# Attention, gated convolution FFN and mixing FFN in one program: first tiles' last products moved behind their partners, and four reorderings around them

## The reference

```python
# attention, per batch and head; cum = cumsum(max(s, 0))
scores = q @ k.T / 8 + minimum(-(cum[:, None] - cum[None, :]), 0), causal
attn = exp(scores - max); attn /= attn.sum() + 1e-9
x = concat_heads(attn @ v)                       # 576 x 512
# first FFN: w_in 512 x 1024, conv_w 3 taps along the sequence, w_out 1024 x 512
h = maximum(x @ w_in, 0)
conv = conv_w[0]*h[s-1] + conv_w[1]*h[s] + conv_w[2]*h[s+1]
x1 = (h * sigmoid(conv)) @ w_out
# mixing: U 576 x 32, V 32 x 576; second FFN: w_ch1 512 x 2048, w_ch2 2048 x 512
u = x1 + (x1.T @ U @ V).T
out = u + maximum(u @ w_ch1, 0) @ w_ch2
```

## Time and profile before

| | us |
|---|---|
| median of 3 runs (lowest, highest) | 910.75 (907.56, 912.88) |
| the profiled execution, whole | 910.62 |
| its span, first to last instruction | 908.8 |

### The profile page before, as it was taken

The page is one execution under the profiler, slowest core; times in us unless marked ns, Lnnn a source line. Parts: engine busy times, 40 slices in busy tenths (PEclk is TensorE's granted clock), DMA queues, the critical chain, the costliest instruction groups (busy, mean ns, idle before and its releaser), DMA issues.

```text
span 908.8 us, 15655 instructions
## 1 busy us (share of the span) xinstructions
PE 861.6 (95%) x6184; PEld 809.2 (89%) x6184; DVE 468.5 (52%) x984; ACT 372.5 (41%) x709; POOL 50.6 (6%) x105
## 2 busy tenths in 40 slices
PE   4888898989999999999999999999999999999998
PEld 3666888879998999889998999988999999999998
DVE  6788694464445934555344871455323761442222
ACT  2777675554425634544332653444221431221110
POOL 3021000000000000000000000000000000000000
PEclk9999998989999999999999999999999999999999
DMA  7686945636663557336545454435444444274441
GB/s 162 164 228 157 305 141 189 222 73 199 214 209 104 188 167 259 127 106 212 180 152 177 129 172 145 134 100 184 146 145 169 141 174 150 94 240 182 150 175 53
DMA packets 64396, 150.36 MB, mean 165 GB/s; under 512 B 30026, under 2 KB 44362, under 8 KB 51780
## 3 DMA queue, kind: packets, MB, share of 16 engines
q1 hardware_dynamic: 61252, 144.50, 49.4%
q0 software_dynamic: 3072, 4.87, 2.1%
HBM read 119.15 MB, written 30.11 MB: 164 GB/s over the span
## 4 chain that ended last, share of the span: by engine, by line
PE 66%; DVE 13%; issue 10%; ACT 5%; DMA 4%; POOL 1%; SPq 1%; DVEq 0%; ACTq 0%; POOLq 0%
PE psum L1190 18%; PE psum L1192 18%; PE psum L1191 17%; PE psum L1169 5%; DVE work L958 2%; DVE psum L899 2%; PE psum L1116 2%; DVE work L961 2%; DMA few_scratch<-few 2%; PE psum L1148 2%; PE psum L1146 2%; DMA spread_out<-few_scratch 2%; DVE work L956 1%; ACT work L746 1%; DVE ybuf L973 1%
## 5 line engine op out<-in xcount | busy, mean ns | idle before, releaser
L1190 PE MATMUL psum<-r_hl,ring 128*128 128x288 f32 x512 | 153.6, 300 | 3.2 <-DVE r_hl L1001 1.7
L1190 PE MATMUL psum<-uu_hl,ring 128*128 128x288 f32 x512 | 153.2, 299 | 1.5 <-DVE r_hl L1001 1.5
L1192 PE MATMUL psum<-r_hl,ring 128*128 128x288 f32 x512 | 151.2, 295 | 0.0
L1191 PE MATMUL psum<-r_hl,ring 128*128 128x288 f32 x512 | 151.1, 295 | 0.0
L1192 PE MATMUL psum<-uu_hl,ring 128*128 128x288 f32 x512 | 151.0, 295 | 0.0
L1191 PE MATMUL psum<-uu_hl,ring 128*128 128x288 f32 x512 | 150.9, 295 | 0.0
L783 ACT ACTIVATE r_hl<-psum 128x288 fp32r<-128x288 f32 x128 | 52.5, 411 | 188.1 <-PE psum L1192 188.0
L1001 DVE SCALAR_TENSOR_TENSOR r_hl<-psum,r_hl 128x288 fp32r<-128x288 f32 x128 | 58.5, 458 | 134.7 <-ACT r_hl L783 134.6
L1169 PE MATMUL psum<-probs,va 128*65 128x320 f32 (+4 forms) x448 | 109.6, 364 | 6.5 <-ACT probs L694 6.3
L899 DVE CUSTOM_DVE_ANT_0 psum<-psum,key_late 128x512 f32<-128x512 f32 (+4 forms) x160 | 84.9, 564 | 57.1 <-PE psum L1116 56.8
L1190 PEld LDWEIGHTS psum<-r_hl,ring 128*128 128x128 f32 x512 | 96.6, 189 | 5.5 <-DVE u_acc L1013 2.7
(11 more groups left out here) (101 smaller groups left out, 1626.6 us busy)
## 6 DMA issues: line engine op xcount, KB each, us to landing
ring<-w_scratch SPq DMA_DIRECT2D x74, 1024.0 KB, 4.9
w_scratch<-ring SPq DMA_DIRECT2D x24, 1024.0 KB, 6.1
kq_raw<-in_kq_t SPq DMA_DIRECT2D x64, 288.0 KB, 5.0
stage<-in_w_ch SPq DMA_DIRECT2D x16, 512.0 KB, 4.7
spread_out<-few_scratch POOLq DMA_DIRECT2D x32, 144.0 KB, 3.2
...
```

The source lines that it names most:

```text
L1190: pe.matmul(o, hi, m_hi, start=start, stop=False)
L1191: pe.matmul(o, hi, m_lo, start=False, stop=False)
L1192: return pe.matmul(o, lo, m_hi, start=False, stop=stop)
```

## The change

- `first_products`: in the first pair of w_in, of w_out and of the second FFN's up (unit 0), half 0 does all k-tiles but the last, then half 1 does all but its last, then half 0's last (which waits for the last low part), then half 1's last.
- `turn_at`: head 3 of batch 1 has its turning of maxima (`max_transpose`, `max_to_row`) at step 4, not 3, that is behind the first w_out item of batch 0.
- `EVICT_LATE`: in heads whose step 4 holds turn, rank or mix items, ACT takes the head's result out at the step's end, not at its beginning.
- `key_low` and `query_low` one step later in batches 1 to 3.
- `X_SPLIT`, `NORMALISE`: in batches 1 to 3 pairs 0 and 1 are normalised and split later in the batch.
- `invert_few` of the last pair: for batches 1 to 3 at the end of the last attention step (h=7, g=4), not in the next batch's first step or as END's item 2.
- `rank` waits for each turned tile by itself, in the order of their turning.
- `middle_tap`: in the last batch the convolution's middle tap is made by ACT instead of DVE.

```diff
--- before.py
+++ after.py
@@ -253,6 +253,11 @@
         MAXIMA = [{0: (0, 1), 1: (2,)}, {0: (0,), 1: (1,), 2: (2,)}]
         TURN = [3, 3]
 
+        def turn_at(a, h):
+            return TURN[a > 0] + ((a, h) == (1, 3))
         COPIED = H + 2
         ATT_STEPS = [(h, g) for h in range(H) for g in range(GROUPS)]
 
@@ -334,7 +339,7 @@
                   for a in range(1, B)}
         PLAN = {a: spread(BESIDE[a], len(ATT_STEPS) - 6 * (a == 1), 6 * (a == 1), a == 1) for a in BESIDE}
         END = order(B - 1, second(B - 2, UNITS // 2, UNITS)) + flat(second(B - 1, 0, UNITS))
-        END_INVERT, END_NORMALISE, END_SPLIT = 2, 5, {0: NPAIR - 2, 6: NPAIR - 1}
+        END_NORMALISE, END_SPLIT = 5, {0: NPAIR - 2, 6: NPAIR - 1}
         SEQ = [item for a in range(1, B) for item in BESIDE[a]] + END
         AT = {item: at for at, item in enumerate(SEQ)}
 
@@ -433,11 +438,14 @@
         STEPS = [(a, h, g) for a in PLAN for h, g in ATT_STEPS]
         STEP_BEFORE = dict(zip(STEPS[1:], [items for plan in PLAN.values() for items in plan]))
 
-        X_SPLIT = [{(5, 0): 0, (7, 0): 1}, {(4, 0): 0, (6, 0): 1}]
+        EVICT_LATE = {(a, h) for a in PLAN for h in range(H - 1)
+                      if any(x[0] in ("turn", "rank", "mix") for x in PLAN[a][GROUPS * h + GROUPS - 1])}
+        X_SPLIT = [{(5, 0): 0, (7, 0): 1}, {(5, 0): 0, (7, 0): 1}]
         X_SPLIT_LAST = [{}, {(0, 2): (NPAIR - 2,), (1, 0): (NPAIR - 1,)}, {(0, 0): (NPAIR - 2,), (0, 2): (NPAIR - 1,)}]
 
-        NORMALISE = [(4, 6), (3, 5, 7)]
-        INVERT_LAST = [(0, 1), (0, 0)]
+        NORMALISE = [{(4, 2): 0, (6, 2): 1}, {(4, 1): 0, (6, 1): 1, (7, 3): 2}]
         NORMALISE_LAST = [(0, 4), (0, 1)]
 
         def multiplied(eng, item):
@@ -711,12 +719,12 @@
                     act.activation(x_hl[0][:, pair, :], x_raw[:, pair, :], ACT.Copy).then_inc(xh_done.sem, 1)
 
                 def attention_step(a, h, g):
-                    if g == TURN[a > 0]:
+                    if g == turn_at(a, h):
                         max_to_row(a, h + 1)
                     if g == 3 and not a:
                         prepare_keys(a, h + 2)
                         prepare_queries(a, h + 2)
-                    if g == 4:
+                    if g == 4 and (a, h) not in EVICT_LATE:
                         evict_head(a, h)
                     for c in {0: (0, 1), 1: (2,), 2: (3,)}.get(g, ()):
                         exponentials(a, h, c)
@@ -730,6 +738,8 @@
                         prepare_keys(a, h + 2)
                     if g == 3:
                         prepare_queries(a, h + 2)
+                    if g == 4 and (a, h) in EVICT_LATE:
+                        evict_head(a, h)
 
                 def hidden(b, f, half):
                     mm_wi.wait(act, b, 2 * f + half + 1)
@@ -737,6 +747,13 @@
                     act.activation(hid[:, f % 2, 1 + half * HALF:1 + (half + 1) * HALF],
                                    half_at("wi", b, 0, f, half), ACT.Relu)\
                        .then_inc(relu.sem, 1)
+                def middle_tap(b, f):
+                    m = b * FT + f
+                    relu.wait(act, b, 2 * f + 2)
+                    yl_done.wait(act, m - 2)
+                    act.activation(conv[f % 2], hid[:, f % 2, 1:S + 1], ACT.Copy, scale=cw[:, 1, f:f + 1]).then_inc(cv.sem, 1)
 
                 def gate(b, f):
                     cv.wait(act, b * FT + f)
@@ -812,6 +829,8 @@
                     kind, b, unit, i, half = item
                     if kind == "wi":
                         hidden(b, i, half)
+                        if half and b == B - 1:
+                            middle_tap(b, i)
                         if i and not half:
                             gate(b, i - 1)
                     if kind == "gated":
@@ -836,6 +855,7 @@
                     if g == 1 and h in WEIGHTS_HEADS:
                         weights_high(MADE[WEIGHTS_HEADS.index(h)])
                 act.wait_ge(s_hid, 1)
+                act.wait_ge(cw_in, 48)
                 bodies(body_step, ffn_step, then)
                 follow(PLAN[B - 1][-1][-1])
                 for x, item in enumerate(END):
@@ -934,16 +954,18 @@
                         query_low(a, h + 2)
                     if g == 3 and h in (2, 4, 6):
                         invert_few(a, h // 2 - 1)
-                    if g == 2 + (a > 0) and h in NORMALISE[a > 0]:
-                        normalise_few(a, NORMALISE[a > 0].index(h))
-                    if g == 2 and a:
+                    if (h, g) in NORMALISE[a > 0]:
+                        normalise_few(a, NORMALISE[a > 0][h, g])
+                    if g == 3 and a:
                         key_low(a, h + 2)
-                    if g == 3 and a:
+                    if g == 4 and a:
                         query_low(a, h + 2)
                     if (a, h, g) == (1, 0, 1):
                         normalise_few(0, NPAIR - 2)
-                    if a and (h, g) == INVERT_LAST[a > 1]:
-                        invert_few(a - 1, NPAIR - 1)
+                    if (a, h, g) == (1, 0, 1):
+                        invert_few(0, NPAIR - 1)
+                    if a and (h, g) == (H - 1, 4):
+                        invert_few(a, NPAIR - 1)
                     if a and (h, g) == NORMALISE_LAST[a > 1]:
                         normalise_few(a - 1, NPAIR - 1)
 
@@ -953,7 +975,8 @@
                     yl_done.wait(dve, m - 2)
                     if f < 2 and b:
                         acc.wait(dve, b - 1, 2 * f + 2)
-                    dve.tensor_scalar(conv[i], hid[:, i, 1:S + 1], cw[:, 1, f:f + 1], None, ALU.mult).then_inc(cv.sem, 1)
+                    if b < B - 1:
+                        dve.tensor_scalar(conv[i], hid[:, i, 1:S + 1], cw[:, 1, f:f + 1], None, ALU.mult).then_inc(cv.sem, 1)
                     cv.wait(dve, m, 1)
                     dve.scalar_tensor_tensor(out=conv[i], in0=hid[:, i, 0:S], scalar=cw[:, 0, f:f + 1], in1=conv[i],
                                              op0=ALU.mult, op1=ALU.add).then_inc(cv.sem, 1)
@@ -1074,8 +1097,6 @@
                 dve.wait_ge(cw_in, 48)
                 bodies(attention_step, ffn_step, then)
                 for x, item in enumerate(END):
-                    if x == END_INVERT:
-                        invert_few(B - 1, NPAIR - 1)
                     if x == END_NORMALISE:
                         normalise_few(B - 1, NPAIR - 1)
                     if x in END_SPLIT:
@@ -1178,7 +1199,7 @@
                         max_transpose(a, h + 1)
                     if g >= 1:
                         values(a, h, g - 1)
-                    if g == TURN[1] and a:
+                    if g == turn_at(a, h) and a:
                         max_transpose(a, h + 1)
                     if g in (1, 2):
                         scores(a, h, g + 1)
@@ -1214,26 +1235,37 @@
                     if kind == "down":
                         acc.wait(pe, b, NTH[item] + 1)
 
-                def products(item, tiles, m_hi, m_lo, ready=None):
+                def products(item, tiles, m_hi, m_lo, ready=None, ks=None):
 
                     half = item[-1]
                     hi, lo = weights(item)
-                    for k in range(tiles):
+                    for k in ks or range(tiles):
                         if ready:
                             ready(k)
                         mm = three(half_at(*item), hi[:, k, :], lo[:, k, :], m_hi[:, k, cols(half)], m_lo[:, k, cols(half)],
                                    k == 0, k == tiles - 1)
                     return mm
 
+                def first_products(item, tiles, m_hi, m_lo, ready):
+                    if item[-1] == 0:
+                        other = (*item[:-1], 1)
+                        products(item, tiles, m_hi, m_lo, ready, range(tiles - 1))
+                        if BEFORE[other]:
+                            evicted(BEFORE[other])
+                        products(other, tiles, m_hi, m_lo, None, range(tiles - 1))
+                    return products(item, tiles, m_hi, m_lo, ready, range(tiles - 1, tiles))
                 def wi(item):
                     _, b, _, f, half = item
                     x_ready = lambda k: xl_done.wait(pe, b * NPAIR + k)
-                    products(item, KT, *x_hl, x_ready if f == 0 and half == 0 else None).then_inc(mm_wi.sem, 1)
+                    (products(item, KT, *x_hl) if f else first_products(item, KT, *x_hl, x_ready)).then_inc(mm_wi.sem, 1)
 
                 def wo(item):
                     _, b, _, d, half = item
                     y_ready = lambda k: yl_done.wait(pe, b * FT + k)
-                    products(item, FT, *y_hl, y_ready if d == 0 and half == 0 else None).then_inc(mm_wo.sem, 1)
+                    (products(item, FT, *y_hl) if d else first_products(item, FT, *y_hl, y_ready)).then_inc(mm_wo.sem, 1)
 
                 def turn(b, t, half):
 
@@ -1247,12 +1279,16 @@
 
                 def rank(b, half):
 
-                    x1l.wait(pe, b)
```

(15 more changed lines are left out.)

## The result

| | before | changed |
|---|---|---|
| median (lowest, highest), us | 910.06 (907.56, 912.88), 6 runs | 899.29 (897.76, 901.21), 6 runs |
| the profiled execution, whole | 910.62 | 898.22 |
| its span | 908.8 | 896.4 |
| its mean granted clock of PE | 0.992 | 0.996 |

The ratio is 0.9882 with a 95% interval of 0.9855 to 0.9909: the changed kernel is 1.2% faster. The forecast was 898.0 with a range of 893.5 to 903.5.

A forecast was written before the change was run, and what follows sets the result against it. PE, busy 95% of the span, was taken as the bound, so gains come from its waits: 5.8 + 1.4 + 2.0 + 1.5 + 1.95 = 12.65 us off 910.6 gives 898, range 893.5 to 903.5.

The forecast's parts named there:

- First w_out, 5.8: Batch 0's first w_out pair: turning behind 42 matmuls at full clock, ending at 144.6 instead of 150.4, 5.8 us gained.
- the rival in which the first w_out gains nothing: Last `y_low` as late as PE was, clock still falls: 5.8 shrinks to 1, total 906, chance 5%.
- Net 0.2 earlier: Batch 0's w_in: covered stall of 0.96 less 0.76 for a query's low part, so the last `y_low` comes 0.2 us earlier.
- my 0.76: A query's low part moved into DVE's dense w_in stretch: 0.76 us cost, also taken off twice in later batches.
- Rank, 1.4: Batch 0's rank at 182.56: its 1.7 us wait for the last two turned tiles shrinks, 1.4 us gained.
- Heads of w_in, 1.34, 1.83 and 1.3: Stalls for x's last low part at the w_in heads of batches 1, 2 and the last one go entirely.
- Late eviction, 1.4 and 0.46: Beside the next batches: relu no longer behind head 3's evict, removing PE stalls of 1.4 and 0.46 us.
- End, 0.65: Last w_in: tap on ACT cuts the period from 3.65 to 3.5, taking 0.65 us off the stall at 739.50.
- The 2.6 us for the 6.9 us at 139.5: First low-clock stretch, in batch 0's first w_out item: 2.6 us lost on 24 matmuls, counted as regained.
- two clock rivals: Clock falls elsewhere or the first stretch stays: 901, 12%. Second low stretch goes too: 895, 13%.
- the slower rival, SP's queue: Raw key and query loads delay ring loads queued behind: 0.7 for each of 23 heads gives 914, chance 4%.
- DVE's backlog: Rival: gains at the heads of stages return as longer waits for the maxima, 902, chance 15%.

The follow-up runs named there:

- e1: The kernel before with only head 3's turning of maxima moved behind the first w_out item: 910.28 us, ratio 1.0026.
- e3: The kernel before with both the moved turning of head 3's maxima and `first_products`, no other edit: 903.45 us, ratio 0.9946.
- e6: The changed kernel with the heads' results taken out at the beginning of step 4 everywhere, as before: 901.09 us, ratio 0.9932.
- e2: The kernel before with `first_products` alone: 907.82 us, ratio 0.9982.
- e5: The changed kernel with low parts of keys and queries back at their old steps: 899.44 us, ratio 0.9907.
- e11: e10 with low parts back at old steps in heads 0 to 2 of batch 1 and for head 0's query in batches 2 and 3: 894.31 us.
- e8: The changed kernel with rank waiting once for all turned tiles, in the old order: 898.66 us, ratio 0.9898.
- e7: The changed kernel with the last pair's inversion back where it was before: 905.05 us, ratio 0.9955.
- e4: The changed kernel with the last batch's middle tap back on DVE: 899.28 us, ratio 0.9893.
- e10: The changed kernel with turning of maxima of heads (2,1) and (3,1) also at step 4, and the middle tap back on DVE: 901.94 us, ratio 0.9919.
- e12: The changed kernel word for word, run again on the same chip as three of its variants: 900.57 us, ratio 0.9913.

## Why the prediction was right, and where it was not

Set against the ledger, the sum of 12.65 stands so (first relu rows to last, profiled against profiled, 12.4 us):

| stretch | predicted gain, terms | measured |
|---|---|---|
| up to batch 0's third relu | 0.96 | 1.5 |
| D | -0.76 | -2.0 |
| A | (5.8 - 0.2) + 1.4 + 1.34 = 8.34 | 8.7 |
| B | 1.4 - 0.76 + 1.83 = 2.47 | 2.5 |
| C | 0.46 - 0.76 + 1.3 = 1.0 | 2.0 |
| end | 0.65 | -0.2 |

The 8.7 in A agree with 8.34 by some luck. A of before has 10.24 us more of low clock, at 0.39 worth 4.0 us, and the sum had only the 2.6 of the first stretch; so the code brought 4.7 where the sum had 5.7. By places (start of the pair's, the rank's last matmul): 5.8 up to the end of the first w_out pair (150.36 and 145.06; the sum 5.6), 1.1 more up to the rank's end (187.52 and 181.16; the sum 1.4), 1.8 more up to batch 1's w_in (the sum 1.34), of which 1.3 are the second low stretch, half as long.

**First w_out, 5.8.** Right as a mechanism and as a number: 42 matmuls unbroken, the last `y_low` done at 143.1 (forecast 142.5), half 1's end at 145.2 (forecast 144.6), full clock there. The absolute times fit by some luck, since the trace was ahead by 1.5 us at the third relu and then lost 2.0 in D. e1 and e3 show that neither move does it alone; the rival in which the first w_out gains nothing is what e1 measured.

**Low parts in batch 0's w_in: mis-sized.** The step that failed is "Net 0.2 earlier", 0.96 for the covered stall less 0.76 for one query's low part. The 0.96 came: from PE's wait for the exponentials in front of w_in (92.38 in before, 92.75 in e6, both at full clock behind it) to the third relu are 9.29 us before and 8.28 in e6, and D is the same 33.2 in before and in e2, so PE's lead is kept. But the low parts cost 2.0 in D, not 0.76 (e5, e11 and every run of the table by its setting). D holds four of them in either kernel, but behind 110, where DVE hardly pauses, stand three now (112.2, 128.1, 131.0) and two before (123.2, 128.7): that is my 0.76. The rest is where they stand: PE waits 1.0 us longer for the maxima of 120.03, which the move put behind more work of DVE. I had priced the length of the piece and not who waits behind it; which of the three costs how much was not tested. What helped the sum is that the later step brings 1.8 back in A, of which I had only the 0.6 of the key's low part. In batches 2 and 3, where I took off 0.76 twice, that cost came, 1.0 and 0.8 in the w_in stretches (e5), but not as the longer wait for maxima that I named: at 304.27 it is 0.64, as at 311.45 before, and the 0.81 at 295.96 is new. What I had at nothing, the other low parts, brings 0.9 and 0.7 behind them, and so B and C come out the same with either setting.

**Rank, 1.4.** The size is about right, 1.0 to 1.3 from the late eviction (e6) and 0.4 from the waits by tile (e8) when each is undone, 1.1 for the whole change between the w_out pair and the rank's end. My "exponentials come some 0.3 later" is the new wait at 189.43; it is 0.4 longer than the mix's wait that it stands in for. That wait of 1.20 (195.41), like the 1.55 at 92.38, contradicts my sentence that the stalls left out are shorter than 1.1 us and that the change touches none: with the low parts in their old places it is back (1.21 in e5).

**Heads of w_in, 1.34, 1.83 and 1.3.** The waits went, but the reason given was half wrong. I wrote that nine matmuls lie in front as well, and costed the evictions of half 1's bank at nothing. e2, e3 and e7 show that in batches 1 and 2 `first_products` alone only changes the name of the wait (in the last it took 1.16 off C), and that without the earlier inversion the changed kernel is 5.8 us slower. What removes the wait is that DVE no longer stands long in front of its evictions: it waits 0.27 and 0.49 for the spread DMA of the last pair, where it was 2.26 and 2.75 before and is 2.17 and 2.74 in e7. In the last batch the reciprocal stands 17.1 us ahead of the third relu, 14.9 before: 2.2 sooner, not 3.5, and enough.

**Late eviction, 1.4 and 0.46.** B's size came (1.50 in e6) but only a third of it where I put it: at 368.57 e6 waits 0.85, the changed kernel still 0.33 at 367.45; e6 loses 0.4 more behind that and 0.6 at the head of batch 2's w_in. C was too small (1.07). I had priced only the one stall that named it, at 591.09; e6 has two in that stretch, 0.30 and 0.25 of idle time or 0.46 and 0.41 as stalls (starts 582.82 and 624.58).

**End, 0.65: wrong in sign.** The loop was drawn rightly, its link from ACT to DVE was too short. ACT's groups by line from 694 to 740 (mean ns is the second number), then the loop in ACT's and DVE's timelines:

```profile
L756 ACT ACTIVATE work<-hid,cw 128x576 f32<-128x576 f32 x8 | 6.2, 778 | 0.3
L763 ACT ACTIVATE work<-work 128x576 f32<-128x576 f32 x8 | 5.5, 686 | 8.1 <-DVE work L984 8.1
```

```profile
711.52 0.69 ACT L763 ACTIVATE work<-work 128x576 f32<-128x576 f32 x1 [0.96 <-DVE work L984]
712.11 0.40 ACT L747 ACTIVATE hid<-psum 128x288 f32<-128x288 f32 x1
712.54 0.78 ACT L756 ACTIVATE work<-hid,cw 128x576 f32<-128x576 f32 x1
```

```profile
709.82 0.82 DVE L981 SCALAR_TENSOR_TENSOR work<-hid,cw,work 128x576 f32<-128x576 f32 x1 [0.45 <-ACT work L756]
...
713.45 0.82 DVE L981 SCALAR_TENSOR_TENSOR work<-hid,cw,work 128x576 f32<-128x576 f32 x1 [0.45 <-ACT work L756]
```

Tanh to relu 0.59, relu to tap 0.43, tap to DVE's next tap 0.91 (713.45 - 712.54: 0.78 and 0.13 of hand-over), two taps 1.70: 3.63, where I had 0.69 for the tap's link and 3.5 in sum. The period before was 3.65. So nothing is won a tile, and the first tile's tap comes 0.4 later (0.91 for 0.51): e4, e10 and e11 all have 0.2 to 0.25 less at the end. The Trainium skill (ScalarE: Activation LUTs, What ACT_TABLE_LOAD costs) says that each per-partition operand of an activation adds about 93 ns; the rows agree, 778 against 686 ns, and I had not used it.

**The clock.** The 2.6 us for the 6.9 us at 139.5 agree with what A shows for the same code, 0.39 us for each us at the lower level. By the Trainium skill (TensorE: Matmul & The Clock Gate, HAM oscillation) it would be half of the length, an estimate of 3.4 for 6.83; the runs give 2.66. That part of such a stretch is idle or paced by others is my reading and was not tested. Of the two clock rivals each came half true: the second low stretch shrank by half, and a short one stood at 90.5. The Trainium skill's other rule (the same page, A second HAM failure mode), that frequent short idles suffice, fits the place, for behind 100 us no idle time longer than 1.6 us precedes the fall at 189.5; but the same short idles did not always bring a fall, see the last section.

**Medians and one execution.** The pair of traces differs by 12.4 us, the medians by 10.8; the trace had a head start by chance. Its wait for the exponentials in front of w_in stands at 90.28, in before at 92.38, in all fourteen traces at 90.3 to 93.9 (e12, the same kernel, at 91.86), with no edit that explains these. Of the 2.1 us, with the stall's 1.0 added, the low clock at 90.5 took 1.5 back, which leaves the 1.5 of the first row. The forecast's 898.0 lies within the changed kernel's runs, but its errors (D and the end against the head start, the clock in A and C) cancelled in it. No matmul waits for a ring load (PE's table of waits has no row for one), so the slower rival, SP's queue, did not come; DVE's backlog came as the 2.0 in D and the 1.0 and 0.8 in the next two w_in stretches. The later normalising of pairs 0 and 1 and the reordered first pair of `up` had no run of their own, so that they cost nothing is not shown.
